# Attention and two networks on one core: probabilities transposed by VectorE and regrouped by transfers in SBUF, x1 normalised later

## What is computed

```python
kv_pool = kv.reshape(B, H // 4, 4, W // 4, 4, C).mean(axis=(2, 4))   # B=2, H=384, W=32, C=128
k = v = kv_pool.reshape(B, -1, C) @ w_sr                             # 768 keys a batch
s = (q @ k.transpose(0, 2, 1)) / np.sqrt(C)                          # q: 2 x 12288 x 128
a = np.exp(s - s.max(-1, keepdims=True))
a /= a.sum(-1, keepdims=True) + 1e-09
x1 = (a @ v).reshape(B * 12288, C)
h = x1 @ moe_w_in;  x2 = (h * np.cos(h)) @ moe_w_out                 # d_ff = 2048
h = x2 @ moe2_w_in; y = (h / (1 + np.exp(-1.702 * h))) @ moe2_w_out
```

## Time and profile before

| what | value |
|---|---|
| median of three runs | 2651.97 us |
| span of the profiled execution | 2650.0 us |
| TensorE busy, matmuls | 2642.2 us (100%), 12551 |
| VectorE busy | 2174.3 us (82%) |
| ScalarE busy | 1929.0 us (73%) |
| GpSimd busy | 2038.4 us (77%) |
| transfers' share of 16 DMA engines | 11.0% |
| mean matmul of 512 columns in the networks | 389 ns |

### The profile page before, as it was taken

The page is one execution under the profiler, slowest core; times in us unless marked ns, Lnnn a source line. Parts: engine busy times, 40 slices in busy tenths (PEclk is TensorE's granted clock), DMA queues, the critical chain, the costliest instruction groups (busy, mean ns, idle before and its releaser), DMA issues.

```text
span 2650.0 us, 40918 instructions
## 1 busy us (share of the span) xinstructions
PE 2642.2 (100%) x12551; PEld 2213.6 (84%) x12551; DVE 2174.3 (82%) x2786; ACT 1929.0 (73%) x2502; POOL 2038.4 (77%) x1900
## 2 busy tenths in 40 slices
PE   9999999999999999999999999999999999999999
PEld 8888888888888888888888888888888888888887
DVE  8999899987778787878787878787888888787876
ACT  5777777787777777777777777777777777777776
POOL 4887677579787878888878787878887878787873
PEclk9999999999999999999999999999999999999999
DMA  7323222200000000000000000000000000000000
GB/s 204 72 48 97 61 48 48 52 21 13 8 16 8 16 9 15 15 9 16 8 16 8 16 8 16 8 16 8 16 8 16 8 16 8 16 8 16 11 10 13
DMA packets 217397, 67.66 MB, mean 26 GB/s; under 512 B 200336, under 2 KB 201488, under 8 KB 216336
## 3 DMA queue, kind: packets, MB, share of 16 engines
q1 hardware_dynamic: 216304, 67.07, 11.0%
q10 hardware_dynamic: 1056, 0.13, 0.0%
HBM read 42.01 MB, written 25.17 MB: 25 GB/s over the span
## 4 chain that ended last, share of the span: by engine, by line
PE 99%; DVE 0%; DMA 0%; ACT 0%; SPq 0%; issue 0%
PE psum L644 29%; PE psum L645 29%; PE psum L646 29%; PE psum L691 7%; PE psum L848 5%; DMA kv_all<-in_kv 0%; PE psum L746 0%; DVE kv_all L1136 0%; DVE g_lo L1308 0%; PE psum L728 0%; PE psum L762 0%; PE psum L661 0%; DVE kv_all L1139 0%; PE psum L668 0%; ACT g_hi L1078 0%; PE psum L735 0%
## 5 line engine op out<-in xcount | busy, mean ns | idle before, releaser
L629 POOL TENSOR_TENSOR g_lo<-g,g_hi 128x512 fp32r<-128x512 f32 x768 | 1132.8, 1475 | 62.3 <-ACT g_hi L1085 2.2
L1308 DVE TENSOR_TENSOR g_lo<-g,g_hi 128x1024 fp32r<-128x1024 f32 (+1 forms) x396 | 666.8, 1685 | 413.9 <-ACT g L1080 413.9
L1078 ACT ACTIVATE g_hi<-psum 128x1024 fp32r<-128x1024 f32 (+1 forms) x396 | 397.3, 1003 | 557.3 <-PE psum L646 557.3
L626 POOL CAST g_hi<-g 128x512 fp32r<-128x512 f32 x750 | 503.8, 672 | 341.7 <-DVE g L1299 341.7
L644 PE MATMUL psum<-x_hi,w_lo 128*128 128x512 f32 x1536 | 597.9, 389 | 0.0
L644 PE MATMUL psum<-g_hi,w_lo 128*128 128x512 f32 x1536 | 597.7, 389 | 0.1
L646 PE MATMUL psum<-x_hi,w_hi 128*128 128x512 f32 x1536 | 597.6, 389 | 0.0
L645 PE MATMUL psum<-x_lo,w_hi 128*128 128x512 f32 x1536 | 597.5, 389 | 0.0
L646 PE MATMUL psum<-g_hi,w_hi 128*128 128x512 f32 x1536 | 597.5, 389 | 0.0
L645 PE MATMUL psum<-g_lo,w_hi 128*128 128x512 f32 x1536 | 597.5, 389 | 0.0
L1299 DVE TENSOR_TENSOR g<-psum,g 128x512 f32<-128x512 f32 x768 | 489.7, 676 | 1.9 <-ACT g L1071 1.8
(11 more groups left out here) (104 smaller groups left out, 2779.0 us busy)
## 6 DMA issues: line engine op xcount, KB each, us to landing
x_dram<-x_out SPq DMA_DIRECT2D x48, 256.0 KB, 2.0
x_raw<-x_dram SPq DMA_DIRECT2D x48, 256.0 KB, 2.7
out<-y_blocks SPq DMA_DIRECT2D x190, 64.0 KB, 2.3
q_blocks<-in_q SPq DMA_DIRECT2D x184, 64.0 KB, 2.2
kv_all<-in_kv SPq DMA_DIRECT2D x6, 1024.0 KB, 9.7
kv_all<-in_kv SPq DMA_DIRECT2D x4, 1536.0 KB, 12.0
w_raw<-in_moe_w_in SPq DMA_DIRECT2D x2, 1024.0 KB, 4.9
q_blocks<-in_q SPq DMA_DIRECT2D x2, 256.0 KB, 5.1
```

Of the source, the lines that this page charges most:

```text
L626: nc.gpsimd.tensor_copy(g1_hi[at][:, t], g1[at][:, t]).then_inc(g1_hi_ready, 1)
L629: nc.gpsimd.tensor_tensor(g1_lo[at][:, t], g1[at][:, t], g1_hi[at][:, t].bitcast(F32), ALU.subtract).then_inc(g1_lo_ready, 1)
L1078: nc.scalar.activation(g2_hi[ring2(j, p)][:, t], h2[buffer2(j)][:, t], ACT.Silu, scale=GELU)
L1308: nc.vector.tensor_tensor(g2_lo[ring2(j, p)][:, t], g2[ring2(j, p)][:, t], g2_hi[ring2(j, p)][:, t].bitcast(F32), ALU.subtract).then_inc(g ...
```

## The change

The probabilities are no longer transposed by TensorE. VectorE transposes each tile's 128x768 in 32x32 blocks into `turned` (`turn`), four tiles side by side. When a chunk's four tiles are there, SyncE issues 16 DMAs from SBUF to SBUF (`regroup`, each 32 partitions x 6 x 128 columns) that bring the blocks to their partitions in `gathered`. ScalarE rounds a chunk in three parts of 128x1024 (`round_probabilities`, slot 8 on), GpSimd makes the low parts (`lower_probabilities`; VectorE the last four), and TensorE sums values from slot 9 on: in three slots of four the products with the rounded part of a third, then those with the low part.

The probabilities aren't multiplied by the inverse sum. The inverse of each chunk goes to DRAM (`save_inverse`), comes back spread over 128 partitions, and GpSimd multiplies x1 by it in the networks (`round_x1`). The queries come in rows by one DMA and are transposed by TensorE, as the first two chunks were. Batch 1 is loaded in rows and pooled by TensorE, two matmuls a slot in 48 slots (`pool_late_rows`). The weights are loaded in two pieces at a time; ScalarE rounds and GpSimd subtracts them in 16 pieces of 512 columns, one each fourth slot. The loops are written out for all 192 tiles. The core of the diff:

```diff
+    TILES = B * SB
+    KEY_BLOCKS = KEYS // BLK
+    GROUPS = P // BLK
+    PARTS = 3
+    PART_TILES = KT // PARTS
+    HI_SLOT, VALUES_SLOT, STORE_SLOT = 8, 9, 15
+    POOL_SLOT, POOL_SLOTS, POOL_GAP = 20, 16, 18
+    WP_COLS = 512
+    PIECES_A_WEIGHT = F // WP_COLS
+    WEIGHT_PIECES = 4 * PIECES_A_WEIGHT
+    WEIGHT_ORDER = (3, 0, 1, 2)
+    UNSCALE_SLOT, SPLIT_SLOT, SPLIT_GAP = 84, 106, 4
+    KEY_SLOTS = {SB - 6: 2, SB - 5: 3, SB - 2: 4, SB: 5}
+    REGROUPED = GROUPS * GROUPS * 16
+    LAST_LO = [(CHUNKS - 2, PARTS - 1)] + [(CHUNKS - 1, i) for i in range(PARTS)]
...
+            def load_queries(c):
+                sp.wait_ge(q_transposed, 1 if c == 2 else c)
+                sp.dma_start(q_blocks[:, :].rearrange("p (s c) -> p s c", c=C),
+                             q_rows[c]).then_inc(q_loaded, 16)
+            def regroup(c):
+                b, n = c // CB, c % 2
+                sp.wait_ge(turned_made, (c + 1) * SUB)
+                if c >= 3:
+                    sp.wait_ge(values_summed, c - 2)
+                if c == CB + 1:
+                    sp.wait_ge(piece_made, 4)
+                src = turned[b][n][:, :, :].rearrange("p (k f) t -> p k f t", f=GROUPS)
+                for a in range(GROUPS):
+                    for f in range(GROUPS):
+                        sp.dma_start(
+                            gathered[b][c % 3][f * BLK:(f + 1) * BLK, :, a * P:(a + 1) * P],
+                            src[a * BLK:(a + 1) * BLK, :, f, :]).then_inc(regrouped[n], 16)
+            def save_inverse(c):
+                n = c % 2
+                sp.wait_ge(inverse_ready, c + 1)
+                sp.dma_start(inverse_dram[c].rearrange("(j p) -> p j", p=P),
+                             inverse[:, n * SUB:(n + 1) * SUB],
+                             allow_slow_non_contiguous=True).then_inc(inverse_saved[n], 16)
...
+            for c in range(CHUNKS):
+                if c + 3 < CHUNKS:
+                    load_queries(c + 3)
+                if c < HT * SUB:
+                    load_late_rows(c)
+                if c == 18:
+                    sp.wait_ge(part_copied, HT)
+                    load_weight(0)
+                    load_weight(1)
+                if c == 31:
+                    load_weight(2)
+                if c == 35:
+                    load_weight(3)
+                regroup(c)
+                save_inverse(c)
+                if c >= 3:
+                    save_x1(c - 3)
+                if c == CHUNKS - 4:
+                    sp.wait_ge(w_split, WEIGHT_PIECES)
+                    for n in range(2):
+                        sp.wait_ge(x1_saved[n], 16)
+                        sp.wait_ge(inverse_saved[n], 16)
+                        load_x1(n, n)
+            for c in range(CHUNKS - 3, CHUNKS):
+                save_x1(c)
...
-            def scale(s, p):
-                j = p % SUB
-                pool.wait_ge(inverse_ready, s + 1)
-                nc.gpsimd.tensor_tensor(probs[p % 4][:, :], probs[p % 4][:, :],
-                                        inverse[:, j:j + 1].to_broadcast([P, KEYS]),
-                                        ALU.mult).then_inc(probs_ready, 1)
...
+            def lower_probabilities(c, i):
+                b, t = c // CB, part_tiles(i)
+                pool.wait_ge(probs_hi_ready, c * PARTS + i + 1)
+                nc.gpsimd.tensor_tensor(probs_t_lo[b][c % 3][:, t, :], gathered[b][c % 3][:, t, :],
+                                        probs_t_hi[c % 2][:, t, :].bitcast(F32),
+                                        ALU.subtract).then_inc(probs_lo_ready, 1)
...
-                pool.wait_ge(x1_loaded[n], 16 * loads)
+                pool.wait_ge(x1_loaded[n], 32 * loads)
+                nc.gpsimd.tensor_tensor(x1_raw[n][:, :], x1_raw[n][:, :], x1_inv[n][:, :],
+                                        ALU.mult).then_inc(x1_scaled, 1)
+                pool.wait_ge(x1_scaled, c + 1)
...
+            for s in range(VALUES_SLOT, TILES):
+                c, i = divmod(s - VALUES_SLOT, SUB)
+                if i < PARTS:
+                    lower_probabilities(c, i)
+                if (s - UNSCALE_SLOT) % 2 == 0 and 0 <= s - UNSCALE_SLOT < 2 * PIECES_A_WEIGHT:
+                    unscale_piece((s - UNSCALE_SLOT) // 2)
+                if (s - SPLIT_SLOT) % SPLIT_GAP == 0:
+                    i = (s - SPLIT_SLOT) // SPLIT_GAP
+                    if 0 <= i < WEIGHT_PIECES:
+                        split_piece(i)
+                if s == TILES - 8:
+                    round_x1(0, 0, 1)
+                if s == TILES - 4:
+                    round_x1(1, 1, 1)
+            for i in range(2):
+                lower_probabilities(CHUNKS - 2, i)
             def split_g1(i, p):
...
+            def sum_upper(c, i):
+                b = c // CB
+                if i == 0:
+                    if c == 0:
+                        pe.wait_ge(v0_split, 4)
+                    if c == CB:
+                        pe.wait_ge(piece_lo_ready, 4)
+                    if c >= 2:
+                        pe.wait_ge(x1_ready, c - 1)
+                pe.wait_ge(probs_hi_ready, c * PARTS + i + 1)
+                for t in range(KT)[part_tiles(i)]:
+                    nc.tensor.matmul(x1_ps[c % 2], v_lo[b][:, t, :], probs_t_hi[c % 2][:, t, :],
+                                     start=t == 0, stop=False)
+                    nc.tensor.matmul(x1_ps[c % 2], v_hi[b][:, t, :], probs_t_hi[c % 2][:, t, :],
+                                     start=False, stop=False)
+            def sum_lower(c, part):
+                b = c // CB
+                for t in part:
+                    if t % PART_TILES == 0:
+                        i = t // PART_TILES
+                        if (c, i) in LAST_LO:
+                            pe.wait_ge(last_lo_ready, LAST_LO.index((c, i)) + 1)
+                        else:
+                            pe.wait_ge(probs_lo_ready, c * PARTS + i + 1)
+                    last = nc.tensor.matmul(x1_ps[c % 2], v_hi[b][:, t, :],
+                                            probs_t_lo[b][c % 3][:, t, :],
+                                            start=False, stop=t == KT - 1)
+                if t == KT - 1:
+                    last.then_inc(values_summed, 1)
+            def sum_values(c, step):
+                if step < PARTS:
+                    sum_upper(c, step)
+                if step == PARTS - 1:
+                    sum_lower(c, range(1))
+                if step == PARTS:
+                    sum_lower(c, range(1, KT))
...
-                    pe.wait_ge(probs_ready, s + (b * SB + 1))
-                    for h in range(2):
-                        if not (b == 0 and static and s == 0):
-                            pe.wait_ge(probs_lo_ready, s * 2 + (b * SB * 2 - 1 + h))
-                        for t in range(KH):
-                            k = (h * KH + t) * P
-                            last = nc.tensor.transpose(probs_ps[h][:, t * P:(t + 1) * P],
-                                                       probs[p % 4][:, k:k + P], ident[:, :])
-                        last.then_inc(probs_transposed, 1)
...
+            for s in range(TILES):
+                if s + 2 < TILES:
+                    next_score(s + 2)
+                else:
+                    i = s + 2 - TILES
+                    if i == 0:
+                        pe.wait_ge(w_split, WEIGHT_PIECES)
+                    pe.wait_ge(exp_done, TILES - 1 + i)
+                    up1(i, i, 0)
+                if s >= VALUES_SLOT:
+                    sum_values(*divmod(s - VALUES_SLOT, SUB))
+                if s % SUB == 2 and s // SUB + 2 < CHUNKS:
+                    next_queries(s // SUB + 2)
+                t, m = divmod(s - POOL_SLOT, POOL_GAP)
+                if 0 <= t < HT and m < POOL_SLOTS:
+                    pool_late_rows(t * POOL_SLOTS + m)
+                if s in KEY_SLOTS:
...
+            sum_values(CHUNKS - 3, PARTS)
+            for i in range(PARTS):
+                sum_upper(CHUNKS - 2, i)
             up1(2, 2, 0)
-            sum_values(B - 1, CHUNKS - 1, 3, 8, x1_last_ps)
+            sum_lower(CHUNKS - 2, range(KT))
+            for i in range(PARTS):
+                sum_upper(CHUNKS - 1, i)
             up1(3, 3, 0)
-            sum_values(B - 1, CHUNKS - 1, 8, 3 * KT, x1_last_ps)
+            sum_lower(CHUNKS - 1, range(KT))
...
+            def round_probabilities(c, i):
+                b, t = c // CB, part_tiles(i)
+                if i == 0:
+                    act.wait_ge(regrouped[c % 2], REGROUPED * (c // 2 + 1))
+                    if c >= 2:
+                        act.wait_ge(values_summed, c - 1)
+                nc.scalar.activation(probs_t_hi[c % 2][:, t, :], gathered[b][c % 3][:, t, :],
+                                     ACT.Copy).then_inc(probs_hi_ready, 1)
...
+            for s in range(TILES - 1):
+                if s + 2 < TILES:
+                    exponentials(s + 2)
```

(62 more changed lines are left out.)

695 lines of the change are left out of this document (267 added, 428 removed).

## The result

The changed kernel takes 2956.8 us (four runs, 2953.2 to 2963.8) against 2651.9 (four runs, 2651.9 to 2652.0): a ratio of 1.1153, 95% interval 1.1137 to 1.1168, or +305 us. The direction was forecast, the size was not: 2659 was predicted, 2643 to 2700 as the range.

The account below looks back on a forecast made before the run. It took a circle of score, maximum, exponential, rounding and values as the bound, 10.75 us a chunk against 10.95. Loop -2, drain +8 and x1 +1 gave +7 on 2650.0, plus 1.97: 2659 us, range 2643 to 2700.

Parts of the forecast that it names:

- 19 issues are 9.1 us: SyncE's queue, per chunk: sixteen transfers, query load, inverse and x1, at 0.48 us an issue taken from q.
- the circle: Attention loop: score, maximum, exponential, rounding, values close over two slots; 4.26 us to the rounded third, 10.75 a chunk.
- The inverse's store: SyncE's queue: 512 elements of 4 bytes a chunk, counted only as one of 19 issues.
- TensorE's own 8.80: TensorE's work in an attention chunk, 8.80 us once probability transposes go and query transposes come.
- GpSimd 2.40: Each GpSimd subtraction of 128x1024 takes 2.40 us undisturbed, up to 2.96.
- Rival 2: Attention: TensorE stays the bound if rounding runs ahead of the exponential; 94 us less, 2565 us; chance 0.05.
- Pooling: Batch 1 on TensorE: two matmuls in each of 48 slots, 0.30 us a slot; 7 us on the circle.
- Chunks that split weights: In 16 chunks an extra GpSimd piece delays TensorE; 0.3 us each reaches the circle, 5 us in all.
- The drain: End of attention: last values 21.2 us after slot 190 instead of 13.2, so +8 us.
- Rival 3: Attention: transfers set the pace, 2681 us, or 2950 if bytes count at both SBUF ends; chance 0.17.
- the sign that was set: Test for transfers setting the pace: the waits before TensorE end with DMA.
- Rival 4: Attention: the clock falls as TensorE idles 18%; at half the clock 17.6 us a chunk, +330 us; chance 0.03.

Follow-up runs that it names:

- e1: The changed kernel with each chunk's inverse sums stored as 128 pieces of 16 bytes instead of 512 of 4 bytes; 2752.5 us.
- e5: e1 with four transfers over 128 partitions in place of sixteen over 32, the regrouping by key left out; 2686.8 us.
- e6: e5 with the rounding of a third placed ahead of the exponential in each of ScalarE's slots; 2618.9 us.
- e13: The changed kernel with only the first of each partition's four inverses stored, 128 pieces of 4 bytes a chunk; 2909.4 us.
- e9: e1 with ScalarE's rounding ahead of its exponential and each regrouping transfer moving 32 rows of 3,072 bytes; 2732.4 us.
- e10: e9 with three of each chunk's sixteen transfers (eight of the last chunk's) issued by ScalarE's queue; 2662.5 us.

## Why the prediction was wrong, step by step

**SyncE's queue (wrong, and the first cause).** "19 issues are 9.1 us" took 0.48 from the moves of q. A regrouping transfer takes 0.606 to issue and 0.65 with its gap, so sixteen are 10.3 and the whole is 12.0 us, above the circle's 10.75. With 0.65 in its place SyncE would have been the bound already on paper: 45 x 1.25 = 56 us more. Taking it away gave 66 (e1 to e5). The prediction bounded the unmeasured terms of VectorE, ScalarE and GpSimd, but not this one, although its row came from another pattern of transfer.

**The inverse's store (wrong, 204 us).** It was counted as one of 19 issues and nothing else. No row of the trace of before showed a 4-byte store, and the term was bounded from neither side. The sentence named "512 elements of 4 bytes" and went on. In the trace such a store lands in 10.2 us and holds up what lies behind it; in 16-byte pieces the 204 us are gone.

**The circle (right, but masked).** 4.26 us predicted, 4.22 and 4.42 found in e5; 10.75 a chunk predicted, 10.92 in e5, and the longer lap is the difference. TensorE's own 8.80: 8.77 in e6. Block transpose 0.97: 0.968. Rounding 1.04: 1.047. GpSimd 2.40: 2.388; it sided with the undisturbed rows. Rival 2, the rounding running ahead, is e6. Its 2565 kept the small sums for pooling, weights and keys, which cost more where TensorE is the bound: in e6 a chunk with pooling is 1.8 us longer than a plain one, and one that splits weights 1.6. That is most of the 54 us by which e6 is above it.

**Smaller terms.** Pooling: two matmuls a slot are four rows in the trace, and so 0.36 + 0.08 us, not 0.30; a pooling chunk is on average 11.63 - 10.92 = 0.7 longer in e5 (0.6 predicted), but 10.60 - 8.77 = 1.8 in e6, where TensorE is the bound. Chunks that split weights: +0.9 in e5, 0.3 predicted. With keys, 2.4 and 4.4 us in two chunks instead of 3.5 in all. Together with the circle's 0.17 x 45 these are 22 of the 25 us by which e5's loop is longer than the sum had it.

**The drain.** 21.2 us predicted; e5 22.7, e6 21.7, the change 38.7, of which one wait of TensorE is 9.89 us and ends with the last rounding. The networks, +1 predicted, +1.2 found.

**Rival 3, transfers set the pace (right in the symptom, wrong in the mechanism).** VectorE's waits ended with DMA (103 us of 400), and through them ScalarE's and TensorE's; TensorE's own row names ScalarE's `probs_t_hi`, so the sign that was set, a wait before TensorE that ends with DMA, shows only at two removes. But neither 188 GB/s (the regrouping reached 286) nor a double count of the bytes was the cause.

**Rival 4, the clock.** "At half the clock" did not come; a share of it did. The granted clock is 0.83 in 100:500 of the change, 0.97 in e1. TensorE's timeline of the change after the long wait of the drain shows both levels:

```profile
852.04 0.77 PE L705 MATMUL psum<-probs_t_hi,v_lo 128*128 128x512 f32 x1 [9.89 <-ACT probs_t_hi L977]
852.60 0.63 PE L707 MATMUL psum<-probs_t_hi,v_hi 128*128 128x512 f32 x1
853.03 0.63 PE L705 MATMUL psum<-probs_t_hi,v_lo 128*128 128x512 f32 x1
...
855.70 0.40 PE L707 MATMUL psum<-probs_t_hi,v_hi 128*128 128x512 f32 x1
855.93 0.39 PE L705 MATMUL psum<-probs_t_hi,v_lo 128*128 128x512 f32 x1
```

After 9.9 us of idleness matmuls start 0.43 us apart, the 1.2 GHz level, and after 855.5 0.23, the 2.4 GHz level. Some 7 matmuls at 0.20 extra are 1.4 us. How much of the 204 us of the small stores comes by way of the clock was not separated. An estimate of its upper bound: in 100:500 a matmul of the change is busy 273.12/1266 = 0.216 us, one of e1 323.56/1603 = 0.202; over the 798 us of the loop that is some 35 us, if all of it held up the end.

## What to carry to other kernels

Count the issues of a queue by a row of the same pattern of transfer, and treat the queue as an engine with a sum of its own: here it was the bound by 1.25 us a chunk, and the row of another transfer hid it. A transfer of a few KB is not cheap if its pieces are 4 bytes: lay the data out so that a partition's numbers are stored in one piece. When a term is taken away and little comes back, look for the next bound beneath: here four lay on one another (16.7, 12.7, 11.4, 10.0 us a chunk), and the same edit was worth 3 us over one and 68 over the other.

## What the runs showed of the hardware that I had not expected

- A store to DRAM in pieces of 4 bytes lands in 10.2 us with 512 pieces (the change) and 9.2 with 128 (e13), and x1's store behind it in 10.8 and 10.1; in 128 pieces of 16 bytes it lands in 1.7 (e1) and x1's in 3.3.
- A regrouping transfer costs SyncE 0.59 us to issue with 32 pieces, 0.61 with 192 and 0.70 with 768 (medians of e9, e1 and e5); x1's and q's cost it 0.44 and 0.43.
- Transfers over 32 partitions each, in flight together, moved 286 GB/s (the change, 316:318).
- An issue by ScalarE's queue, 0.61 us, runs while its engine computes, and three a chunk cost the engine little (e9 to e10, 70 us gained); with six, its roundings stood idle 16.3 us of 400.
